# Loads of units 0 and 1 from two queues, gap rows loaded, every second reciprocal, a second scores buffer

## The reference

```
for t in range(S):                          # RWKV-like recurrence, per batch and head
    cur = einsum('bhd,bhe->bhde', u * k[t], v[t])
    y[t] = einsum('bhd,bhde->bhe', r[t], state + cur)
    state = w[t][..., None] * state + einsum('bhd,bhe->bhde', k[t], v[t])
x = y as (3072 tokens, 384)
x = relu(x @ w_in) ** 2 @ w_out             # 384 -> 2048 -> 384
do = (x @ w_skip) > 0                       # tokens that go on to the experts
e = argmax(x @ w_gate), p = softmax at e    # 8 experts, one per token
out = x;  out[do] += p * (relu(x @ w1[e]) @ w2[e])   # 384 -> 1024 -> 384
```

## Time and profile before

| | |
|---|---|
| median of 3 runs | 761.67 us (761.53 to 762.62) |
| profiled execution, its own time | 761.0 us |
| its span, first to last instruction | 759.4 us |
| TensorE matmul busy | 738.6 us (97%) |
| VectorE, ScalarE, GpSimd busy | 475.6, 305.2, 231.1 us |
| granted TensorE clock | 0.996 of full speed |

### The profile page before, as it was taken

The page is one execution under the profiler, slowest core; times in us unless marked ns, Lnnn a source line. Parts: engine busy times, 40 slices in busy tenths (PEclk is TensorE's granted clock), DMA queues, the critical chain, the costliest instruction groups (busy, mean ns, idle before and its releaser), DMA issues.

```text
span 759.4 us, 15493 instructions
## 1 busy us (share of the span) xinstructions
PE 738.6 (97%) x5808; PEld 665.1 (88%) x5808; DVE 475.6 (63%) x767; ACT 305.2 (40%) x601; POOL 231.1 (30%) x213
## 2 busy tenths in 40 slices
PE   6899999999999999999999999999999999999995
PEld 3578888888988888888988889899999999999894
DVE  8988887866676666866577645434652326635871
ACT  3655534434333334433443333253241114524841
POOL 7753423212242221411242220245251112312311
PEclk9999999999999999999999999999999999999998
DMA  9886224221133223322231205154466116616710
GB/s 242 249 263 190 69 64 143 68 63 40 42 114 71 63 64 105 95 63 63 45 116 46 62 34 187 47 175 156 157 208 241 63 53 212 226 53 214 245 31 14
DMA packets 51073, 88.35 MB, mean 116 GB/s; under 512 B 6668, under 2 KB 34424, under 8 KB 50992
## 3 DMA queue, kind: packets, MB, share of 16 engines
q1 hardware_dynamic: 42240, 61.21, 28.5%
q0 software_dynamic: 7648, 24.51, 8.9%
q10 hardware_dynamic: 1104, 1.57, 0.6%
HBM read 72.79 MB, written 16.95 MB: 118 GB/s over the span
## 4 chain that ended last, share of the span: by engine, by line
PE 92%; DVE 2%; DMA 2%; issue 1%; POOL 1%; ACT 1%; SPq 0%; DVEq 0%; POOLq 0%; ACTq 0%
PE bank L637 27%; PE bank L639 26%; PE bank L638 26%; PE bank L704 3%; PE bank L749 2%; PE bank L733 2%; PE bank L779 1%; PE bank L869 1%; DMA x<-w_out_t 1%; PE bank L713 1%; PE bank L738 1%; PE bank L743 1%; ACT spare L1042 1%; PE bank L952 1%; DMA odds<-u_rows 1%
## 5 line engine op out<-in xcount | busy, mean ns | idle before, releaser
L637 PE MATMUL bank<-wo_hi,h_hi 128*128 128x394 f32 (+1 forms) x536 | 187.0, 349 | 0.0
L637 PE MATMUL bank<-xt_hi,wi_hi 128*128 128x512 f32 (+1 forms) x528 | 183.1, 347 | 0.0
L639 PE MATMUL bank<-wo_hi,h_lo 128*128 128x394 f32 (+1 forms) x536 | 182.7, 341 | 0.0
L638 PE MATMUL bank<-wo_lo,h_hi 128*128 128x394 f32 (+1 forms) x536 | 182.3, 340 | 0.0
L638 PE MATMUL bank<-xt_lo,wi_hi 128*128 128x512 f32 (+1 forms) x528 | 180.0, 341 | 0.0
L639 PE MATMUL bank<-xt_hi,wi_lo 128*128 128x512 f32 (+1 forms) x528 | 179.9, 341 | 0.0
L1456 DVE SCALAR_TENSOR_TENSOR hid<-bank,hid 128x512 f32<-128x512 f32 x96 | 65.3, 680 | 123.4 <-ACT hid L1080 123.2
L1080 ACT ACTIVATE hid<-bank 128x512 f32<-128x512 f32 x96 | 57.1, 595 | 165.0 <-PE bank L639 158.1
L1722 POOL TENSOR_TENSOR work<-work 112x512 f32<-112x512 f32 x24 | 35.7, 1486 | 248.7 <-DVE work L1271 246.6
L639 PEld LDWEIGHTS bank<-xt_hi,wi_lo 128*128 128x128 f32 x528 | 100.1, 190 | 11.9
L637 PEld LDWEIGHTS bank<-xt_hi,wi_hi 128*128 128x128 f32 x528 | 100.0, 189 | 10.1 <-issue 0.2
(11 more groups left out here) (176 smaller groups left out, 1020.9 us busy)
## 6 DMA issues: line engine op xcount, KB each, us to landing
work<-rkw SPq DMA_DIRECT2D x48, 192.0 KB, 4.1
spare<-rk_rows SPq DMA_DIRECT2D x22, 384.0 KB, 4.5
work<-sorted_rows SPq DMA_DIRECT2D x24, 193.0 KB
work<-rkw SPq DMA_DIRECT2D x48, 96.0 KB, 3.4
work<-v_rows SPq DMA_DIRECT2D x24, 192.0 KB, 4.0
work<-w POOLq DMA_DIRECT2D x6, 768.0 KB, 5.8
x<-w POOLq DMA_DIRECT2D x6, 768.0 KB, 7.4
out<-x SPq DMA_DIRECT2D x20, 192.0 KB
```

Source lines behind the costliest of these rows:

```text
L637: pe.matmul(ps, a_hi, b_hi, start=start, stop=False, skip_group_check=True)
L638: pe.matmul(ps, a_hi, b_lo, start=False, stop=False, skip_group_check=True)
L639: return pe.matmul(ps, a_lo, b_hi, start=False, stop=stop, skip_group_check=True)
```

## The change

Parts of the diff that follows, in its order: the second scores buffer (`scores_of`: odd units of chunk 0 use a free half of `hid` and the tail of `stage[1]`); the loads of units 0 and 1, halves 0 from SP and halves 1, u and the own rows of unit 1 from ScalarE, without a wait for a memset; half 0 now loads 64 rows, so that the gap holds rows of the other head, and no memset of ones is made; SP's list in a new order, `early_decays` waiting for the reciprocals and piece 2 for `ps_att`; TensorE's low-part products of f = 0 and 1 both ahead of the wait for the last token rows; `inverse` as a reciprocal of every second step and one multiplication for the others (1/cum[t-1] = w[t]/cum[t]); a new order of steps on VectorE in the start; experts of odd number take their single tile first.

```
+        def scores_of(c, b, half):
+            if c == 0 and b % 2:
+                ap = (hid[:, 0, :], stage[1][:, SECOND:SECOND + PAIRS * T])[half]
+                return ap.rearrange("p (j t) -> p j t", j=PAIRS)
+            return scores[:, half]
...
+        def rows_of(half):
+            return (slice(0, HALF), slice(HALF, HALF + D))[half]
+        def source_of(unit, half):
+            return rkw[bass.ds(unit, 1)].rearrange("x h p n -> (x h p) n")[(slice(0, HALF), slice(D, 2 * D))[half]]
+        def decays_in(engine, unit, half):
+            engine.dma_start(by_time(w_dec[unit % 2])[rows_of(half), :, 1:T + 1],
+                             source_of(unit, half)[:, RK:].rearrange("p (j t) -> p j t", j=PAIRS)
+                             ).then_inc(decay_loaded[unit % 2], 16)
+        def rk_into(engine, unit, half):
+            engine.dma_start(rk_in[unit % 2][rows_of(half)].rearrange("p a j t -> p (a j t)"),
+                             source_of(unit, half)[:, 0:RK]).then_inc(loaded[unit % 2], 16)
+        def own_into(engine, c, b):
+            engine.dma_start(own_of(c, b), rk_rows[bass.ds((B * c + b) % UNITS, 1)].rearrange("x t d -> (x t) d")
+                             ).then_inc(own_loaded[b % 2], 16)
...
             def load_mlp_piece(k):
                 elif k == 2:
-                    sp.wait_ge(own_summed, B)
+                    sp.wait_ge(ps_att, B)
             def early_decays(unit):
-                sp.wait_ge(cum_done, unit - 1)
+                sp.wait_ge(inv_done, 2 * unit - 2)
...
+                if i == 0 and f == 0:
+                    for early in range(2):
+                        for k in range(KD):
+                            pe.matmul(HID[early][:, 0:2 * T], wi_lo[:, k, early * T:early * T + T],
+                                      xt_hi[0][:, k, 0:2 * T], start=False, stop=(k == KD - 1),
+                                      skip_group_check=True)
                 if f == 0:
                     pe.wait_ge(sb_xlo, B * i + B)
...
-                keep_busy((1, 4, 1, 0)[b])
+                keep_busy((1, 3, 2, 0)[b])
...
             def own_diagonal(c, b):
-                if unit > 0:
+                if c > 0:
                     act.wait_ge(ps_att, unit)
+                elif b > 1:
+                    act.wait_ge(ps_att, unit - 1)
...
+            decays_in(act, 0, 1)
+            rk_into(act, 0, 1)
+            act.dma_start(own_u[:, :], u_rows).then_inc(u_loaded, 16)
+            decays_in(act, 1, 1)
+            rk_into(act, 1, 1)
+            own_into(act, 0, 1)
...
             def inverse(c, b, part):
-                two = slice(part * PAIRS // 2, (part + 1) * PAIRS // 2)
-                dve.reciprocal(inv_of(c, b)[0:PK, :].rearrange("p (j t) -> p j t", j=PAIRS)[:, two],
-                               by_time(cum[b % 2])[0:PK, two, 1:T + 1]).then_inc(inv_done, 1)
+                steps = inv_of(c, b)[0:PK, :].rearrange("p (j t two) -> p j t two", j=PAIRS, two=2)
+                n = b % 2
+                if part == 0:
+                    dve.reciprocal(steps[:, :, :, 1], by_time(cum[n])[0:PK, :, 2:T + 1:2]).then_inc(inv_done, 1)
+                else:
+                    dve.wait_ge(inv_done, 2 * unit + 1)
+                    dve.tensor_tensor(steps[:, :, :, 0], steps[:, :, :, 1], by_time(w_dec[n])[0:PK, :, 2:T + 1:2],
+                                      ALU.mult).then_inc(inv_done, 1)
...
-            for b in range(2):
-                factors(0, b, own_first=True)
+            for b in range(2):
+                factors(0, b)
             own_rows(0, 2)
             receptance(0, 2)
             keys(0, 2)
             factors(0, 3, own_first=True)
+            pool.wait_ge(w_lo, 1)
             own_rows(1, 0)
...
             def expert(e, p, begin, pairs, singles, singles_end):
+                if e % 2:
+                    with pe.If(singles < singles_end):
+                        single_item(e, p, begin, singles)
+                    with pe.If(begin < pairs):
+                        with pe.Fori(begin, pairs) as q:
+                            pair_item(e, p, q, singles_end)
```

More of the change, by code:

```diff
@@ L649, in layer1 @@
                 cols = slice(f * T, f * T + T)
-                if i == 0 and f < 2:
-                    for k in range(KD):
-                        pe.matmul(HID[f][:, 0:2 * T], wi_lo[:, k, cols], xt_hi[0][:, k, 0:2 * T], start=False,
-                                  stop=(k == KD - 1), skip_group_check=True)
                 tokens = slice(2 * T if i == 0 and f < 2 else 0, B * T)
@@ L1038, in own_diagonal @@
                 act.wait_ge(own_summed, unit + 1)
-                if unit > 0:
+                if c > 0:
                     act.wait_ge(ps_att, unit)
+                elif b > 1:
+                    act.wait_ge(ps_att, unit - 1)
                 for h in range(H):
-                    last = act.activation(scores[:, h % 2, h // 2, :], ident[:, :], ACT.Copy,
+                    last = act.activation(scores_of(c, b, h % 2)[:, h // 2, :], ident[:, :], ACT.Copy,
                                           scale=own_sum[:, b % 2, h:h + 1])
@@ L1212, in expert, with splits @@
                 more = e + 1 if e + 1 < NE else None
-                with act.If(begin < pairs):
-                    pair_item(begin, singles)
+                def splits():
                     if more is not None:
@@ L1217, in expert @@
                             split_expert_hi(k, more)
-                with act.If(begin + 1 < pairs):
-                    with act.Fori(begin + 1, pairs) as q:
-                        pair_item(q, singles)
-                with act.If(singles < singles_end):
+                if e % 2:
+                    with act.If(singles < singles_end):
+                        single_item(begin, singles, more)
                     with act.If(begin < pairs):
-                        single_item(pairs, singles)
-                    with act.If(begin >= pairs):
-                        single_item(pairs, singles, more)
+                        pair_item(begin, singles_end)
+                        with act.If(singles >= singles_end):
+                            splits()
+                    with act.If(begin + 1 < pairs):
+                        with act.Fori(begin + 1, pairs) as q:
+                            pair_item(q, singles_end)
+                else:
+                    with act.If(begin < pairs):
+                        pair_item(begin, singles)
+                        splits()
+                    with act.If(begin + 1 < pairs):
+                        with act.Fori(begin + 1, pairs) as q:
+                            pair_item(q, singles)
+                    with act.If(singles < singles_end):
+                        with act.If(begin < pairs):
+                            single_item(pairs, singles)
+                        with act.If(begin >= pairs):
+                            single_item(pairs, singles, more)
                 if more is not None:
@@ L1228, in expert @@
                         act.wait_ge(e_y, begin * 2 + singles + 1)
-                        for k in range(PIECES):
-                            split_expert_hi(k, more)
+                        splits()
             for n in range(GROUPS):
@@ L1292, in mask_scores @@
                 dve.sem_inc(waits_held_dve, 1)
-                dve.copy_predicated(scores[:, half, :, :],
+                dve.copy_predicated(scores_of(c, b, half),
                                     before[:, :].bitcast(I32).unsqueeze(1).to_broadcast([T, PAIRS, T]),
```

151 lines of the change are left out of this document (71 added, 80 removed).

## The result

The changed kernel takes 766.32 us (median of 8 runs, 764.73 to 768.14) against 762.38 us of the kernel before on the same chip (761.38 to 764.52): ratio 1.0052, interval 1.0038 to 1.0066. It is slower by 3.9 us, outside the predicted range.

The account below looks back on a forecast made before the run. The prediction took the start, a chain over loads, GpSimd and VectorE, as what counts, most else hidden under TensorE. Start -2.1, near 98 us -0.3, experts +0.3: -2.1, so median 759.6 us, range 757.5 to 761.9.

Parts of the forecast that it names:

- Part 1: Start up to the mask of unit 2: its r and k land at 20.3, so the mask begins at 27.7, 0.45 sooner.
- landing after 21.5: Sign of being wrong: r and k of unit 2 landing before 19 or after 21.5 us.
- The sum of unit 3 ahead of the mask: Before unit 2's mask, VectorE waits for GpSimd's own rows and takes unit 3's sum, 0.50 us, ending at 25.5.
- rival A: Start gives nothing back: unit 2's load lands at 21.4, GpSimd's own rows take 1.80; 761.5 us, chance 0.28.
- Parts 2 to 4: Unit 2's mask onward: unit 3's mask 0.8 sooner, second layer 2.1 sooner (43.8), layer1(0, 4) still in time at 51.5.
- rival C: Piece 2's load takes 10.0 us and lands at 46.3, so layer1(0, 4) is late: slower, 763.7 us, chance 0.1.
- The gap rows: Start: 320 KB more ahead of unit 2's r and k, 1.1 us later, against a queue filling about 1 us sooner.
- Near 98 us: Chain over a reciprocal: its second half becomes 0.35, 1.4 less, and TensorE's stall goes: -0.3 us.
- The multiplication: New 112 x 256 multiplication on VectorE: 0.37 us by elements, ends 0.3 and 1.0; near 0.35 as a sign.
- Experts: Only expert 3's two items swap; its lone tile carries the splits of expert 4: +0.3 us; the two gaps count 0.
- B: Two queues move more than one: unit 2's load lands 2 to 3 us sooner; 757.2 us, chance 0.08.
- D: Second buffer and early orders do nothing by themselves, as unit 2 is bound by its load; already in the forecast.

Follow-up runs that it names:

- e6: Kernel before with halves 1, u and the own rows of unit 1 issued by ScalarE, 48 rows, memsets and waits kept: 766.02 us, ratio 1.0052.
- e10: Changed kernel with the loads of units 0 and 1, and the orders that go with them, as before: 766.41 us, 1.0060 to the kernel before.
- e13: e10 with the load of piece 0 back ahead of the decays of unit 3 in SP's list: 762.11 us, 1.0010 to the kernel before.
- e11: e10 with the sum and diagonal of unit 3 also at their old places: 763.77 us, 1.0018 to the kernel before.
- e15: e11 with the load of piece 0 ahead of the decays of unit 3: 758.68 us, 0.9963 to the kernel before.
- e3: Kernel before with 64-row instead of 48-row loads of halves 0 alone, memsets kept: 764.22 us, ratio 1.0026.
- e18: e15 with 64 rows in all loads of halves 0 (gap rows): 761.39 us, 1.0000 to the kernel before.
- e8: Kernel before with every second reciprocal, the experts' order and w_out_t ahead of piece 2 in SP's list: 759.40 us, ratio 0.9981.
- e7: Kernel before with the second scores buffer, unit 3's diagonal at its new place and piece 2 waiting for ps_att: 772.11 us, ratio 1.0135.
- e17: Changed kernel with piece 0 ahead of unit 3's decays, and unit 3's sum and diagonal at old places: 765.70 us, 1.0064 to the kernel before.
- e4: Changed kernel with all loads of units 0 and 1 issued by SP in the order of before: 764.87 us, 1.0055 to the kernel before.
- e14: Changed kernel with the load of piece 0 ahead of all waits in SP's list: 764.70 us, 1.0048 to the kernel before.
- e2: Changed kernel with 5 dummy products instead of 1 after the scores of unit 0: 765.24 us, 1.0055 to the kernel before.

## Why the prediction was wrong

**What bounds the kernel.** Right: the start decided. `layer2(0, 0)` came 4.6 us later than before, and of the rest only the experts moved the span, by -0.8.

**Part 1, the step that failed.** "Units 0 and 1 come sooner now": they came 2.8 us later at the scan of unit 1, 3.2 at the mask of unit 0, and 1.7 at the mask of unit 1 (24.14, before 22.49), which I had named as some 3 us sooner. I had priced the two queues as bytes in a full queue with "the order of those bytes is almost the same". That order had changed twice. Two lists interleave, so that what is wanted last delays what is wanted first (e6). And "issued at 16.1, landed 4.2 later, at 20.3" took over both numbers as if fixed. The issue waits for the transposes of unit 0, behind its mask: it came 3.8 us later. The 4.2 held because piece 0 had gone out at 10.03: it became 5.4. In the changed list piece 0 stands behind a wait for the inverse, and so right ahead of r and k (e10 to e13). I had quoted that wait in the change and put no price on it. I named landing after 21.5 as a sign of being wrong; it was 25.36. Of the 6.7 us by which `layer2(0, 0)` missed its forecast (50.48 against 43.8) this step makes 5.1; 0.6 lie between it and the mask of unit 2, 0.3 between the masks of units 2 and 3, and 0.7 behind.

**The sum of unit 3 ahead of the mask.** I named the wait for GpSimd and gave it 25.5 for the end of the sum. The mechanism is there (1.92 us of wait), and GpSimd's own rows took 1.94 and 1.00 where I took twice 1.00; rival A had 1.80. With the early diagonal it costs 2.6 to 3.4 us (e11, e15); I had put 2.5 us of it into the chain as if the mask needed them, and did not ask what the old place would give.

**Parts 2 to 4.** Given their start they held in part. From the mask of unit 2 to that of unit 3 the changed kernel takes 5.97 us where I wrote 5.65 (before: 5.99), so nothing was gained there: its scores waited for GpSimd's k of unit 3, whose load landed at 33.86 and whose multiplication took 2.92. From there to `layer2(0, 0)` it takes 11.15 against 11.73 before, where I wrote 10.45. The wait for w_out_t is gone and piece 1 is split ahead of the key copy, but the last low part stands 3.66 us behind the mask (3.64 before), so the 0.4 us for it did not come. Piece 2 was no bound: its split ended at 57.48 and `layer1(0, 4)` began at 58.16 (rival C did not happen; the slower time has another cause). The forecast for `layer2(0, 0)` was 43.8, and e15, where r and k land at 21.18, starts it at 43.92 and takes 758.68 where I forecast 759.6. That is another kernel, and the agreement is partly luck: its mask of unit 2 comes at 26.41, not 27.7, as the sum of unit 3 stands behind it, and 6.76 us follow to the mask of unit 3, not 5.65.

**The gap rows.** I took 1.1 us for 320 KB and set 1 us against it for the sooner start, which kept 20.3 as landing. That e3 shows 1.1 at the scan of unit 1 is no confirmation: only 128 of the 320 KB lie ahead of it, 0.4 us at 296 GB/s, and SP's last issue for it is 0.9 us later, which I had not priced. At r and k of unit 2 it was 2.3 in e3, and e18 puts 2.7 on the whole.

**Near 98 us.** Wrong, a small term: nothing gained. The chain of the earlier trace rows ran over the first part of the reciprocal (95.90), not the second, and I took the 1.4 off the second. The first part is as long as before, the gate's low part (L1533) waits for it, and the multiplication stands behind both:

```profile
100.55 1.75 DVE L1333 RECIPROCAL odds<-work 112x256 f32<-112x256 f32 x1
102.22 0.63 DVE L1507 SCALAR_TENSOR_TENSOR hid<-bank,hid 128x512 f32<-128x512 f32 x1
102.76 0.18 DVE L1533 TENSOR_TENSOR wo_lo<-bank,wo_hi 128x40 fp32r<-128x40 f32 x1
102.87 0.41 DVE L1336 TENSOR_TENSOR odds<-odds,work 112x256 f32<-112x256 f32 x1
```

**The multiplication** takes 0.43 us (0.35 to 0.37 forecast): right. **Experts:** one issue gap went (1.4 to 0.4), a sum of -0.8 instead of +0.3, inside the bounds given. e8, with the same order of the experts, has the same 0.8 to 0.9 behind `layer2(0, 0)`.

**The rivals.** C was slower by another cause. None had this one: B (two queues move more) is refuted by e6. D ("do nothing by themselves") holds up to the mask of unit 2 (e7: 27.68 against 28.15) and is wrong behind it, where e7's diagonal and moved wait cost 10.4 us. That two lists and a moved wait would make the same bytes arrive in a worse order was in no rival. The scan and GpSimd's multiplication at times take twice as long in the same kernel, and the traces show when: in the changed kernel the scan takes 1.23 us at 5.67 and 12.60, where GpSimd stands idle, and 2.56 at 26.29, beside GpSimd's k and own rows of units 2 and 3; GpSimd's k takes 1.26 at 26.50 and 2.92 at 35.01, beside VectorE's split of 35.06. When one of the two is slowed and when the other, and why, is not shown. Open too: what each of e15's kept parts gives alone, how e17's 7.0 us divide between two lists, 64-row loads and the order of the engines, and what the low clock adds.

## What to carry to other kernels

When loads compete for full DMA engines, their order is the schedule: for each late load ask what it waits for, what stands ahead of it in its list, and when that went out, before you take over its landing time. In this kernel a wait put in front of a large load moved it to where it collided with the next urgent one (e10), or held an urgent one behind it (e7); look first whether large loads can stand ahead of waits, and urgent ones ahead of both. And when one fix alone gains nothing (e4, e10, e14, e17), a second cause may cover it: make the fixes together before you drop either.

## What the runs showed of the hardware

TensorE's granted clock fell to the lower of its levels (0.50, 1.2 GHz) in the start, behind waits of 2.2 to 3.5 us (changed, e7, e10), though not behind each of them (e14 waited 3.20 us before 35.07, and the window from 35 to 40 is at 1.00): from 20 to 25 us in the changed kernel, behind a wait of 3.54 us and a window with 1.72 of 5 us busy. The next window is at 0.69. The 16 products of a unit's scores took 2.08 us there instead of 1.16:

```profile
18.28 1.01 PE L728 MATMUL bank<-ident,work 112*128 112x112 f32 x4 [3.54 <-DVE spare L1344]
...
21.90 2.08 PE L719 MATMUL bank<-work 48*128 48x128 f32 x16
```

The Trainium skill states the rule on "TensorE: Matmul & The Clock Gate" (Part 1): the clock is throttled unless recent activity releases it. The rows agree. Raising the clock from 20 to 30 us gained 0.1 us at `layer2(0, 0)` (e2). Loads of 64 rows instead of 48 cost 1.1 us at the scan of unit 1 in e3 and 2.5 to 2.7 us in the medians of e3 and e18, and a part of it is issue time: 1.28 us instead of 0.91 for two loads.
